# xk @ w_k by seven block products per quad in place of eight, value tiles between them, gates once per batch

## What is computed

```python
u = x + h.transpose(0, 2, 1)                         # from the token mixer
h2 = np.maximum(u @ w_ch1, 0.0) @ w_ch2              # 512 -> 1536 -> 512
x = u + h2
xk = mu_k * x + (1.0 - mu_k) * x_prev                # x_prev: one token back
xr = mu_r * x + (1.0 - mu_r) * x_prev
k = np.maximum(xk @ w_k, 0.0)                        # 512 -> 1024
v = k * k @ w_v                                      # 1024 -> 512
return 1.0 / (1.0 + np.exp(-(xr @ w_r))) * v
```

## Time and profile before

| | |
|---|---|
| three runs | 487.44, 487.47, 486.76 us |
| the profiled execution | 486.72 us, span 485.0 us |
| chain of waits, by engine | PE 80%, ACT 7%, issue 5%, DVE 3% |
| channel quads (12) | from 114.6 us, 15.65 us each in most |
| last stage | first matmul at 314.84 us, 41.5 us a group, last matmul at 480.67 us |

### The profile page before, as it was taken

The page is one execution under the profiler, slowest core; times in us unless marked ns, Lnnn a source line. Parts: engine busy times, 40 slices in busy tenths (PEclk is TensorE's granted clock), DMA queues, the critical chain, the costliest instruction groups (busy, mean ns, idle before and its releaser), DMA issues.

```text
span 485.0 us, 7909 instructions
## 1 busy us (share of the span) xinstructions
PE 465.2 (96%) x2896; PEld 418.9 (86%) x2896; DVE 298.6 (62%) x672; ACT 227.4 (47%) x475; POOL 149.9 (31%) x155
## 2 busy tenths in 40 slices
PE   4889899999999999999999999999999999999996
PEld 4777777788999999999999999899899889989985
DVE  6799998487766665447545875666635436354511
ACT  5899997455533234322333332355545325244411
POOL 6656774352236533653216643000000000000000
PEclk9999999999999999999999999999999999999999
DMA  5999954410212121212112315410010010001001
GB/s 164 265 223 236 210 125 71 131 43 1 88 45 70 61 86 45 88 46 85 43 69 63 131 43 174 126 49 1 0 65 1 0 43 22 0 1 64 0 0 65
DMA packets 42235, 36.92 MB, mean 76 GB/s; under 512 B 20704, under 2 KB 34528, under 8 KB 42208
## 3 DMA queue, kind: packets, MB, share of 16 engines
q1 hardware_dynamic: 42208, 36.58, 28.4%
HBM read 33.43 MB, written 3.15 MB: 75 GB/s over the span
## 4 chain that ended last, share of the span: by engine, by line
PE 80%; ACT 7%; issue 5%; DVE 3%; DMA 2%; POOL 2%; SPq 0%; ACTq 0%; POOLq 0%; DVEq 0%
PE bank L1238 19%; PE bank L1240 19%; PE bank L1239 19%; PE bank L1371 13%; PE bank L1372 7%; ACT e_sb L646 4%; DMA v<-in_v_dram 2%; ACT qbd L626 2%; PE bank L1218 1%; PE bank L1290 1%; POOL xL L557 1%; ACT kt L634 1%; PE bank L1308 1%; POOL v L499 1%; PE bank L1268 0%
## 5 line engine op out<-in xcount | busy, mean ns | idle before, releaser
L1238 PE MATMUL bank<-ucH,w1H 128*128 128x384 f32 x168 | 56.8, 338 | 0.3 <-DVE c L1081 0.2
L1240 PE MATMUL bank<-ucH,w1L 128*128 128x384 f32 x168 | 56.5, 336 | 0.0
L1239 PE MATMUL bank<-ucL,w1H 128*128 128x384 f32 x168 | 56.4, 336 | 0.0
L770 ACT ACTIVATE rH<-c 128x384 fp32r<-128x384 f32 x36 | 18.9, 526 | 69.0 <-DVE c L1081 69.0
L1240 PE MATMUL bank<-xkH,WkL 128*128 128x384 f32 x128 | 43.1, 337 | 0.0
L1238 PE MATMUL bank<-xkH,WkH 128*128 128x384 f32 x128 | 43.0, 336 | 0.0
L1239 PE MATMUL bank<-xkL,WkH 128*128 128x384 f32 x128 | 43.0, 336 | 0.0
L1157 DVE SCALAR_TENSOR_TENSOR k<-bank,kr 128x384 f32<-128x384 f32 x32 | 17.8, 556 | 33.4 <-ACT kr L820 33.4
L1240 PE MATMUL bank<-WvH,k2L 128*128 128x512 f32 x96 | 37.8, 394 | 0.0
L598 POOL TENSOR_TENSOR w2L<-stg,w2H 128x512 fp32r<-128x512 f32 x24 | 37.5, 1585 | 1.0
L1239 PE MATMUL bank<-WvL,k2H 128*128 128x512 f32 x96 | 37.8, 394 | 0.0
(11 more groups left out here) (142 smaller groups left out, 1207.4 us busy)
## 6 DMA issues: line engine op xcount, KB each, us to landing
stg<-in_moe_w_ch_dram SPq DMA_DIRECT2D x24, 512.0 KB, 3.4
vw<-in_v_dram SPq DMA_DIRECT2D x16, 240.0 KB, 5.5
kn<-in_k_dram SPq DMA_DIRECT2D x8, 384.0 KB, 6.1
qn<-in_q_dram SPq DMA_DIRECT2D x8, 384.0 KB, 7.0
v<-in_v_dram SPq DMA_DIRECT2D x8, 384.0 KB, 5.5
out_dram<-o_sb SPq DMA_DIRECT2D x12, 256.0 KB, 2.0
stg<-in_moe_w_k_dram SPq DMA_DIRECT2D x4, 512.0 KB, 3.5
stg<-in_moe_w_v_dram SPq DMA_DIRECT2D x4, 512.0 KB, 4.2
```

What stands on the lines that cost most here:

```text
L770: act.activation(rH[slot][:, f, half * GR:half * GR + GR], src, ACT.Relu).then_inc(rh_done, 1)
L1238: pe.matmul(dst, wH, mH, start=start, stop=False, **more)
L1239: pe.matmul(dst, wH, mL, start=False, stop=False, **more)
L1240: return pe.matmul(dst, wL, mH, start=False, stop=stop, **more)
```

## The change

The last stage is no longer four groups. xk @ w_k becomes eight more quads, four for each batch (q = 12 to 19, `NKP` = 4), built like the channel quads, and h @ w_ch2 between the products becomes k*k @ w_v: `value` tiles of 128 tokens, three matmuls of 512 columns each, 12 in a quad, of the quad before. Each batch's six accumulators lie in banks 2 to 7. Squares are made on VectorE from SBUF (the first from kr, ScalarE's Relu of bank 0). The mixing of xk for a batch (8 mixes, 4 combinations, 7 splits) is spread over earlier quads: batch 0 in quads 7 to 11, batch 1 in 13 to 15. xr is mixed and split in quads 16 (half of it after the quad) and 17, 18. The gate product with Sigmoid, multiplication and stores comes once for each batch, six tiles alternating between banks 0 and 1: after quad 16's products for batch 0, at the end for batch 1. w_k and w_v are loaded and split twice, once for each batch, w_k by the path of w_ch1 and w_v by that of w_ch2 (so on GpSimd); w_r goes through the third staging tile at quads 15 and 16, its high part on ScalarE, its low part on GpSimd. `wide` and `side` of batch 1 stand inside quad 12.

The diff, cut:

```diff
-    NWT, NFP, NK, NV = 6, FC // 2, FK // 2, FK // 2
+    NWT, NFP, NKP = 6, FC // 2, FK // 2
     NQ = B * NFP
+    NA = NQ + B * NKP
+    NT = 2 * RT
...
+        T_AT = {(1, 0): (3,), (2, 0): (4,), (3, 0): (5,), (4, 0): (6,),
+                (9, 1): (3, 4), (9, 2): (5, 6), (14, 1): (3, 4), (14, 2): (5, 6)}
+        U_AT = {(1, 1): (0,), (2, 1): (1,), (3, 1): (3,), (4, 1): (4,), (4, 2): (5,), (5, 1): (6,), (5, 2): (2,),
+                (10, 1): (0, 1), (10, 2): (3,), (11, 1): (4, 5), (11, 2): (6, 2),
+                (14, 3): (0, 1), (15, 1): (3, 4), (15, 2): (5, 6), (15, 3): (2,)}
+        MIX_AT = {(7, 1): ((0, 0), (1, 0)), (7, 2): ((2, 0), (3, 0)), (8, 1): ((0, 1), (1, 1)), (8, 2): ((2, 1), (3, 1)),
+                  (13, 1): ((0, 0), (1, 0), (2, 0), (3, 0)), (13, 2): ((0, 1), (1, 1), (2, 1), (3, 1))}
+        XR_AT = {(16, 1): (0, 1), (16, 2): (2, 3), (17, 1): (0, 1), (17, 2): (2, 3), (18, 1): (4, 5), (18, 2): (6, 7)}
+        XR_HIGH_AT = {(16, 2): (0, 1), (16, 3): (2, 3), (17, 2): (0, 1), (17, 3): (2, 3), (18, 2): (4, 5), (18, 3): (6, 7)}
+        XR_LOW_AT = {(16, 3): (0, 1, 2, 3), (17, 3): (0, 1, 2, 3), (18, 3): (4, 5, 6, 7)}
...
# SP
+            for q in range(NA):
+                if q + 2 < NA:
                     sp.wait_ge(w1_split, q + 1)
                     load_w1(q + 2)
+                if q < NA - 1:
+                    if q == 16:
+                        wait_piece(sp, "wr", 1)
+                        load_piece("w2", 16)
+                    wait_piece(sp, "w2", q)
+                    if q == 15:
+                        load_piece("wr", 0)
+                        wait_piece(sp, "wr", 0)
+                        load_piece("wr", 1)
+                    else:
+                        load_piece("w2", q + 1)
+                if q == NQ + NKP:
+                    for n in range(NT):
+                        store(n)
...
# GpSimd
+            for q in range(NA):
+                if 1 <= q < NA - 1:
                     sums_w1(q + 1)
+                if q == 16:
+                    low_wr(0)
+                    low_wr(1)
...
# ScalarE
+            def quad_k(q):
+                slot, done, k = q % 2, NPROD * q, q - NQ
+                def high_k(n, f, half, src):
+                    act.wait_ge(sq_done, 4 * k + n)
+                    act.activation(rH[slot][:, f, half * GR:half * GR + GR], src[:, :], ACT.Copy).then_inc(rh_done, 1)
+                act.wait_ge(prod_done, done + P1)
+                act.activation(p1[:, :], bank[0][:, 0:GR], ACT.Copy).then_inc(p1_done, 1)
+                if q == 16:
+                    high_wr(0)
+                ahead(q, 1)
+                act.wait_ge(prod_done, done + P2)
+                act.wait_ge(rl_done, 4 * (q - 1) + R11)
+                act.activation(kr[:, :], bank[0][:, 0:GR], ACT.Relu).then_inc(kr_done, 1)
+                if q < NA - 1:
+                    high_w1(q + 1)
+                wait_second(act, q - 2)
+                high_k(R11, 0, 0, kr)
+                ahead(q, 2)
+                high_k(R22, 1, 1, c22)
+                if q == 16:
+                    high_wr(1)
+                high_k(R21, 1, 0, c21)
+                high_k(R12, 0, 1, c12)
+                ahead(q, 3)
...
+                if q == NQ + 1:
+                    act.wait_ge(x2_done, 6 * B)
+                quad_k(q)
+                if q == NQ + NKP:
+                    for n in range(KT, 2 * KT):
+                        mix_r(0, n)
+                    for n in range(KT, 2 * KT):
+                        high_xr(0, n)
+                    gates(0)
+            gates(1)
...
# VectorE
+                def square(n, c):
+                    dve.wait_ge(sum_done, 5 * q + n + 1)
+                    dve.scalar_tensor_tensor(out=c[:, :], in0=c[:, :], scalar=0.0, in1=c[:, :], op0=ALU.max,
+                                             op1=ALU.mult).then_inc(sq_done, 1)
...
+                plus(P6, u2, Bk, p1)
+                dve.wait_ge(kr_done, k + 1)
+                dve.tensor_tensor(kr[:, :], kr[:, :], kr[:, :], ALU.mult).then_inc(sq_done, 1)
+                ahead(q, 1)
+                if q == NQ:
+                    wide(1, 0)
+                plus(P7, u3, Bk, p1)
+                low_k(R11, 0, 0, kr)
+                if q < NA - 1:
+                    low_w1(q + 1, 0)
+                dve.wait_ge(sum_done, 5 * q + 2)
+                dve.wait_ge(rl_done, 4 * q)
+                plus(P5, c22, A, u3)
+                square(R22, c22)
+                ahead(q, 2)
+                if q == NQ:
+                    wide(1, 1)
+                low_k(R22, 1, 1, c22)
+                plus(P4, c21, Bk, p1)
+                square(R21, c21)
+                if q < NA - 1:
+                    low_w1(q + 1, 1)
+                low_k(R21, 1, 0, c21)
+                if q == NQ:
+                    side(1, 1)
+                plus(P3, c12, A, u2)
+                square(R12, c12)
+                low_k(R12, 0, 1, c12)
+                if q == NQ:
+                    wide(1, 2)
+                    wide(1, 3)
+                    side(1, 3)
+                ahead(q, 3)
...
+                if q == NQ + NKP:
+                    for n in range(KT, 2 * KT):
+                        mix_r(0, n)
+                    for n in range(KT, 2 * KT):
+                        low_xr(0, n)
+                    outputs(0)
+            outputs(1)
...
# TensorE
+            TILE_GAPS = (range(0, 2), range(2, 3), range(3, 5), range(5, 6), range(6, 8), range(8, 10), range(10, 12))
+            for q in range(NA):
                 for n in range(NPROD):
                     product(q, n)
+                    if q > NQ:
+                        for m in TILE_GAPS[n]:
+                            value(q - 1, *TILES[m])
...
+                if q == NQ + NKP:
+                    gate(0)
+            for f, st in TILES:
+                value(NA - 1, f, st)
+            gate(1)
```

More of the change, by code:

```diff
@@ new lines, in mix_r, with low_xr @@
+            def mix_r(b, n):
+                kk, half = n % KT, n // KT
+                dst = xrF[:, kk, half * GR:half * GR + GR]
+                dve.wait_ge(tr_mixed, 8 * b + n + 1)
+                dve.scalar_tensor_tensor(out=dst, in0=u_tile(kk, 2 * b + half), scalar=mu[:, 1, kk:kk + 1], in1=dst,
+                                         op0=ALU.mult, op1=ALU.add).then_inc(xr_mixed, 1)
+            def low_xr(b, n):
+                kk, half = n % KT, n // KT
+                part = slice(half * GR, half * GR + GR)
+                dve.wait_ge(xrh_done, 8 * b + n + 1)
+                dve.tensor_tensor(xrL[:, kk, part], xrF[:, kk, part], xrH[:, kk, part].bitcast(F32),
+                                  ALU.subtract).then_inc(xrl_done, 1)
@@ L1174, in _ @@
[L1174 to L1177 removed]
+            for q in range(NQ, NA):
+                if q == NQ + 1:
+                    dve.wait_ge(x2_done, 6 * B)
+                quad_k(q)
+                if q == NQ + NKP:
[4 more added lines that the diff above has]
+                    outputs(0)
@@ L1377, in second, with value @@
                     ins.then_inc(d_done, 1)
+            def value(q, f, st):
+                k, slot = q - NQ, q % 2
+                first, last_one = first_of_set(q) and f == 1, last_of_set(q) and f == 0
+                if f == 1 and st == 0:
+                    wait_piece(pe, "w2", q)
+                    pe.wait_ge(rl_done, 4 * q + R21)
+                elif f == 0 and st == 0:
+                    pe.wait_ge(rl_done, 4 * q + R12)
+                if first and q == NQ:
+                    pe.wait_ge(x2_done, 6 + (1, 2, 4, 5, 5, 6)[st])
+                elif first:
+                    pe.wait_ge(o_done, st + 1)
+                c, t = slice(f * DM, f * DM + DM), slice(st * P, st * P + P)
+                ins = three(bank[2 + st][:, :], rH[slot][:, f, t], rL[slot][:, f, t], w2H[slot][:, c], w2L[slot][:, c],
+                            first, last_one, skip_group_check=True)
+                if f == 0 and st == NT - 1:
+                    ins.then_inc(v_done, 1)
@@ new lines, in gate @@
+            def gate(b):
+                wait_piece(pe, "wr", 1)
+                for st in range(NT):
+                    if st < 2:
+                        pe.wait_ge(sum_done, 5 * (NQ + NKP + 1 if b == 0 else NA))
+                    else:
+                        pe.wait_ge(sg_done, NT * b + st - 1)
+                    if st % RT == 0:
+                        pe.wait_ge(xrl_done, 8 * b + KT * (st // RT + 1))
+                    t = slice(st * P, st * P + P)
+                    for kk in range(KT):
+                        c = slice(kk % 2 * DM, kk % 2 * DM + DM)
+                        ins = three(bank[st % 2][:, :], xrH[:, kk, t], xrL[:, kk, t], WrH[:, kk // 2, c],
+                                    WrL[:, kk // 2, c], kk == 0, kk == KT - 1)
+                    ins.then_inc(wr_done, 1)
@@ L1437, in _ @@
-            with pe.Fori(0, NGR) as g:
-                last(g)
+                    if q > NQ:
```

(10 more changed lines are left out.)

460 lines of the change are left out of this document (170 added, 290 removed).

## The result

The changed kernel takes 510.82 us (median of 4 runs, 509.05 to 512.30) beside 487.46 for the kernel before on the same chip. The ratio is 1.048, with a 95% interval of 1.044 to 1.052. The forecast was 507.0, range 491 to 513. The profiled execution took 512.3 us, span 510.6.

The account below looks back on a forecast made before the run. It took TensorE's matmuls as the bound, busy 96% of 485.0 us, while other engines keep up. 486.72 - 8.35 - 0.97 + 29.6 of waits (13.1 VectorE alone, 16.5 GpSimd) = 507.0 us, range 491 to 513.

Parts of the forecast that it names:

- What goes: TensorE: 48 hidden-product matmuls fewer (8.35 us) and three waits for VectorE in the channel quads gone (0.97 us): 9.3 us gained.
- VectorE's chain: VectorE's queue in a new quad, up to P3's sum: just fits, 0.15 us to spare, so other late work costs time.
- P4 of quad 12: Quad 12: wide(1, 0) stands ahead of P7's sum, for which P4 waits: 1.5 us of idle TensorE, forced by the order.
- Turns with GpSimd: From quad 9 into the gate: VectorE operations with two SBUF operands and GpSimd's operations wait each other out: 16.5 us.
- gate tile 2: Inside the first gate: the first Sigmoid, with its table load, comes late and this tile waits: 2.0 us.
- Rival 1: VectorE and GpSimd: contention is slight, their waits miss each other; 490.5 us as lower bound, up to 500; chance 0.20.
- VectorE's own waits: Quads 9 to 18 and the first gate: TensorE's waits with VectorE alone, without GpSimd, sum to 13.1 us.
- The clock: TensorE's clock after waits: the forecast's sum held nothing for a fall to half speed.
- rival 3: TensorE's clock falls in the gaps, at the gate and similar waits: 0 to 7 us more, 507 to 514; chance 0.09.
- What would show it: Signs: quads 13 to 16 starting 18 to 20 us apart, waits at c and xrL, gate gap of 5 to 10 us.

Follow-up runs that it names:

- single removals: Changed kernel without, each alone, GpSimd's reading work from quad 12 on (memsets instead), xk's mixing for batch 1, or xr for batch 0: 494.80, 501.01, 501.89 us.

## Why the prediction was right, and where it was off

- **What goes** (9.3 us): held, if a little large. There are 48 matmuls fewer, and where waits were taken away the kernel ended up faster than before. A bare quad takes 15.7 us, where the forecast had 15.52, at most 1.5 us over eight quads that it left out.
- **VectorE's chain** (0.15 us to spare in a bare quad, so that everything else is time): held. Quads 13 to 15 with nothing added had 0.27 to spare. Both ways of giving it room, three operations fewer or the same ones in idle places, were worth 14 to 16 us. The square took 0.56, as its nearest row said.
- **P4 of quad 12** (1.5, forced by the order): 1.50, and 0 once `wide(1, 0)` stood behind P7's sum.
- **Turns with GpSimd** (16.5 us): the mechanism held, and its size roughly. 16.0 us went when GpSimd read nothing, but 3.2 of that is clock, which the forecast didn't have in this term; the waits fell by 14, beside 14.5 in the forecast without gate tile 2. The end less 0.14 gave each length to 0.1 us. Rival 1, slight contention, would have ended at 500 at most.
- **The joint sum.** The forecast added VectorE's own waits (13.1) and the turns (16.5). The single removals overlap by 9 us, so these are shares for this order of removal: most waits had both causes.
- **Gate tile 2** (2.0): this term didn't come, and the clock's fall took its place. Its wait didn't appear because the two tiles ahead ran at the lower clock; with the clock kept up it was there, 1.82.
- **The clock** (nothing in the sum, rival 3 with 0.09): the term that was mis-sized. It fell at three of the waits and cost 6.6 us of TensorE's time instead of 0; rival 3 had this mechanism, with 0 to 7 us. In the profiled execution, which took 5.3 us more than the 507.0, the account closes: 6.6 of clock and 2.4 of the small items above, less 2.0 of gate tile 2 and 1.6 of other waits that were a little shorter, make 5.4. That 507 came so near is in part luck: errors of both signs met, 9.0 us too little and 3.6 too much. How much of it a full clock would give back is less sure: with two of the three falls taken away 2.5 us came back in the profiled execution and 1.0 in the median. At the gate the reason shows, since 1.82 of the 2.2 us came back as the wait of tile 2; why the median moved less than quad 14's 2.7 is open, and the spread of the executions (509.05 to 512.30 for the changed kernel) hides it. The fall behind the start of quad 16 wasn't tried alone.
- **What would show it:** quads 13 to 16 start 19.6, 20.9 and 18.5 us apart (named: 18 to 20), waits stand at c and xrL, and the gate's gap is 9.4: these came. One sign did not: VectorE's operations from SBUF were to take 0.9 us and more in the mean. The squares took 0.65, the low parts of the squares 0.76, and only those of xr 1.17. The turns were long, but met only some of the operations.

## What to carry to other kernels

Before an engine gets work that another engine can't hide, write out its queue against the bound engine's due times: 0.15 us to spare a period meant that 96% busy became 91%. Count two engines that share operand reads as one where their operations overlap late in the period. Where a change that saves matmuls is slower, look for the third engine: ScalarE at 45% took the squares, and with the extras moved to idle places 23 us of loss became 2 to 3 us of gain.
